# Chunked attention beside a bilinear layer: one TensorE visit per chunk, with two array modes in place of four

## The reference, cut to what matters

```python
# 1. gated linear attention; batch 4, heads 8, seq 768, head_dim 48
for t in range(S):
    state = alpha[:, :, t, :, None] * state + np.einsum('bhd,bhe->bhde', k[:, :, t], v[:, :, t])
    y[:, :, t] = np.einsum('bhd,bhde->bhe', q[:, :, t], state)
# 2. bilinear layer, 384 -> 1024 -> 384
x = ((x @ w1) * (x @ w2) @ w3) @ w_out
# 3. four experts, 384 -> 1024 -> 384, weighted by p
p = domain_probs / (domain_probs.sum(-1, keepdims=True) + 1e-09)
for e in range(E):
    out += p[:, e:e + 1] * (np.maximum(x @ w1[e], 0.0) @ w2[e])
```

## Time and profile before

| | |
|---|---|
| median of 3 runs | 1246.04 us (1245.34 to 1248.34) |
| profiled execution, its own time | 1246.21 us |
| its span | 1244.5 us |
| busy PE | 1238.9 us |
| busy DVE | 391.0 us |
| busy ACT | 285.2 us |
| busy POOL | 179.5 us |

### The profile page before, as it was taken

The page is one execution under the profiler, slowest core; times in us unless marked ns, Lnnn a source line. Parts: engine busy times, 40 slices in busy tenths (PEclk is TensorE's granted clock), DMA queues, the critical chain, the costliest instruction groups (busy, mean ns, idle before and its releaser), DMA issues.

```text
span 1244.5 us, 17887 instructions
## 1 busy us (share of the span) xinstructions
PE 1238.9 (100%) x7390; PEld 1119.1 (90%) x7390; DVE 391.0 (31%) x797; ACT 285.2 (23%) x554; POOL 179.5 (14%) x157
## 2 busy tenths in 40 slices
PE   9999999999999999999999999999999999999999
PEld 5699999999999999999999898999999998989998
DVE  4455454544643122222222222122222222222222
ACT  2433333333332421111111111111111111111111
POOL 1522222222222640000000000000000000000000
PEclk9999999999999999999999999999999999999999
DMA  9612323232322431111141111103111111222200
GB/s 280 202 54 87 93 83 106 69 106 69 106 76 94 155 141 51 51 51 51 51 152 52 52 51 51 46 23 135 52 51 51 51 51 51 77 76 76 76 16 36
DMA packets 41314, 99.57 MB, mean 80 GB/s; under 512 B 3360, under 2 KB 13344, under 8 KB 40736
## 3 DMA queue, kind: packets, MB, share of 16 engines
q1 hardware_dynamic: 41248, 98.63, 24.5%
HBM read 82.10 MB, written 14.16 MB: 77 GB/s over the span
## 4 chain that ended last, share of the span: by engine, by line
PE 95%; DMA 2%; DVE 1%; POOL 1%; SPq 1%; issue 0%; DVEq 0%
PE bank L847 30%; PE bank L849 29%; PE bank L848 29%; PE bank L869 2%; PE bank L900 2%; DMA inputs<-akq 1%; PE bank L906 1%; PE bank L882 1%; POOL wb_lo L398 1%; PE bank L856 1%; DMA wo_sb<-w_out 1%; PE bank L990 0%; DVE decay L639 0%; DVE suffix L626 0%; SPq L298 0%; SPq L307 0%
## 5 line engine op out<-in xcount | busy, mean ns | idle before, releaser
L686 DVE SCALAR_TENSOR_TENSOR h_lo<-bank,h_hi 128x512 fp32r<-128x512 f32 x192 | 132.7, 691 | 617.8 <-ACT h_hi L497 617.8
L497 ACT ACTIVATE h_hi<-bank 128x512 fp32r<-128x512 f32 x192 | 115.0, 599 | 663.9 <-PE bank L849 663.9
L848 PE MATMUL bank<-we_lo,h_hi 128*128 128x384 f32 x768 | 257.1, 335 | 0.0
L847 PE MATMUL bank<-we_hi,h_hi 128*128 128x384 f32 x768 | 257.0, 335 | 0.0
L849 PE MATMUL bank<-we_hi,h_lo 128*128 128x384 f32 x768 | 256.9, 335 | 0.0
L849 PE MATMUL bank<-x_hi,we_lo 128*128 128x512 f32 x576 | 228.1, 396 | 0.0
L848 PE MATMUL bank<-x_lo,we_hi 128*128 128x512 f32 x576 | 227.1, 394 | 0.0
L847 PE MATMUL bank<-x_hi,we_hi 128*128 128x512 f32 x576 | 226.4, 393 | 0.0
L847 PEld LDWEIGHTS bank<-we_hi,h_hi 128*128 128x128 f32 x768 | 144.3, 188 | 8.9 <-DVEq L835 0.4
L848 PEld LDWEIGHTS bank<-we_lo,h_hi 128*128 128x128 f32 x768 | 144.1, 188 | 8.8
L849 PEld LDWEIGHTS bank<-we_hi,h_lo 128*128 128x128 f32 x768 | 144.1, 188 | 0.0
(11 more groups left out here) (75 smaller groups left out, 1086.2 us busy)
## 6 DMA issues: line engine op xcount, KB each, us to landing
x_hi<-x_hi_spill SPq DMA_DIRECT2D x24, 768.0 KB, 4.9
x_lo<-x_lo_spill SPq DMA_DIRECT2D x24, 768.0 KB, 6.4
inputs<-akq SPq DMA_DIRECT2D x24, 672.0 KB, 5.6
we_raw<-wset SPq DMA_DIRECT2D x4, 3072.0 KB, 10.2
values<-v_rows SPq DMA_DIRECT2D x24, 256.0 KB, 5.5
x_hi_spill<-x_hi_out SPq DMA_DIRECT2D x8, 576.0 KB, 3.4
x_lo_spill<-x_lo_out SPq DMA_DIRECT2D x8, 576.0 KB, 4.6
w_sb<-w_t SPq DMA_DIRECT2D x16, 256.0 KB, 11.9
```

Of the source, the lines that this page charges most:

```text
L497: act.activation(h_hi[:, s % 2, :], bank[s % 2][:, :], ACT.Relu).then_inc(h_hi_ready, 1)
L686: dve.scalar_tensor_tensor(out=h_lo[:, s % 2, :], in0=bank[s % 2][:, :], scalar=0.0, in1=h_hi[:, s % 2, :], op0=ALU.max, op1=ALU.subtract) ...
L847: pe.matmul(dst, left[0], right[0], start=first, stop=False)
L848: pe.matmul(dst, left[0], right[1], start=False, stop=False)
```

## The change

Per chunk there is now one place on PE at which attention is worked, in the even step (`visit`), instead of two:

- it starts with the value products of chunk c (128x64), then the state products of chunk c+1 (128x64);
- then, in one 64x64 block, the state's share of the outputs of chunk c (`state_share`) mixed with the scores of chunk c+1 (`score`). A score matmul now has 64 keys as weights: the first 64 keys against all 128 queries, the last 64 keys against the last 64 queries only. That is 16 matmuls of 128 or 64 columns where 8 of 128 were;
- the outputs are all in bank 7, so the even heads' share must be complete before the odd heads' share starts (`even_shared`, a wait of PE for itself); the state products are in what is left of banks 5 and 6;
- `mask` is eight operations of 256 or 128 elements instead of two of 512; `add_state` is two instead of one; the x0 split is one instruction of 512 elements instead of two of 256 on ACT and on DVE;
- the preparation of a chunk is done one chunk further ahead, `turn_keys` stands behind `down1` of the odd step, and SP loads a chunk before it moves rows. A copy of the chunk's decay (`chunk_decay`) is added;
- in the start the visits stand at other places, visit 2 (which has the scores of chunk 3) among them; DVE prepares chunk 3 behind `take(0, 1)`, and two of the four parts of the first weight set are loaded after chunk 3's inputs.

```diff
             def mask(b, c):
-                for row in range(2):
-                    dve.tensor_tensor(scores[:, row, :, :], bank[5 + row][:, :]..., causal[:, None, :]..., ALU.mult).then_inc(masked, 1)
+                for row in (1, 0):
+                    dve.wait_ge(scored, 2 * (CHUNKS * b + c) + 2 - row)
+                    # four dve.tensor_tensor: 64 x 2x128, 64 x 2x64, 64 x 2x64, 64 x 2x128
+                last.then_inc(masked, 1)
...
+            def take(b, c):
+                x0_low(b, c)
+                first = chunk_behind(b, c)
+                if first:
+                    if first[1] >= 1:
+                        decay_state(*first)
+                    if first[1] < CHUNKS - 1:
+                        add_state(*first)
+                    mask(*first)
...
+            def state_share(b, c, row, n):
+                g, q = divmod(n, 2)
+                if row == 1 and n == 0:
+                    pe.wait_ge(even_shared, (CHUNKS - 1) * b + c)
+                rows = slice(row * ODD, row * ODD + D)
+                mm = pe.matmul(bank[7][q * ODD:(q + 1) * ODD, (2 * row + g) * CHUNK:(2 * row + g + 1) * CHUNK], decayed[rows, 2 * g + q, :],
+                               inputs[rows, c % SLOTS, Q, 2 * g + q, :], start=False, stop=(row == 1 and g == 1))
+                if n == PAIRS - 1:
+                    mm.then_inc(y_done if row else even_shared, 1)
+
+            def score(c, row, n):
+                pair, half = divmod(n, 2)
+                lower = (pair + half) % 2 == 0
+                at = pair // 2 * GROUP + (pair % 2) * (CHUNK if lower else HALF)
+                rows = slice(row * ODD, row * ODD + D)
+                mm = pe.matmul(bank[5 + row][0 if lower else HALF:HALF if lower else P, at:at + CHUNK - half * HALF],
+                               inputs[rows, c % SLOTS, K, pair, half * HALF:(half + 1) * HALF],
+                               inputs[rows, c % SLOTS, Q, pair, half * HALF:], start=True, stop=True)
...
+            def visit(b, c):
+                value_products(b, c)
+                first = chunk_behind(b, c)
+                if first and first[1] < CHUNKS - 1:
+                    state_products(*first)
+                if first:
+                    wait_scores(*first)
+                if c >= 1:
+                    pe.wait_ge(state_decayed, (CHUNKS - 1) * b + c)
+                if c >= 1 and first:
+                    for n in range(3 * PAIRS):
+                        if n < PAIRS:
+                            state_share(b, c, 0, n)
+                        else:
+                            score(first[1], 0, n - PAIRS)
+                        if n < 2 * PAIRS:
+                            score(first[1], 1, n)
+                        else:
+                            state_share(b, c, 1, n - 2 * PAIRS)
...
                     if chunk and s % 2 == 0:
-                        score(*chunk)
-                        if chunk[1] < CHUNKS - 1:
-                            state_products(*chunk)
-                    if chunk and s % 2:
-                        outputs(*chunk)
-                        if not (last_batch and chunk[1] == CHUNKS - 1) and chunk_behind(*chunk)[1] < CHUNKS - 1:
-                            turn_keys(*chunk_behind(*chunk))
+                        visit(*chunk)
...
                     down1(b, s)
+                    if chunk and s % 2:
+                        second = chunk_behind(*chunk, 2)
+                        if second and second[1] < CHUNKS - 1:
+                            turn_keys(*second)
...
-            first_beside = {3: ((turn_keys, 0),), 4: ((score, 0), (state_products, 0)), 5: ((outputs, 0), (turn_keys, 1)),
-                            6: ((score, 1), (state_products, 1)), 7: ((outputs, 1), (turn_keys, 2))}
-            second_beside = {2: ((score, 2), (state_products, 2)), 6: ((outputs, 2),), 20: ((turn_keys, 3),)}
+            first_beside = {3: (turn_keys, 0), 4: (first_visit, 0), 6: (turn_keys, 1), 7: (visit, 0)}
+            second_beside = {5: (turn_keys, 2), 9: (visit, 1), 15: (turn_keys, 3), 20: (visit, 2)}
...
             pe.wait_ge(fold_lo, FT - 1)
             pe.wait_ge(piece_lo, PIECES)
             up1(0, 0, 1, True)
+            turn_keys(0, 4)
```

More of the change, by code:

```diff
@@ L66 @@
 WARM = 6
-CONSTANTS = 6
+CONSTANTS = 7
 FLAG_STEP = STEPS1 - 4
-PREP_STEPS = 4
+PREP_STEPS = 5
+HALF = CHUNK // 2
+GROUP = 3 * HALF
+STATE_AT = 2 * GROUP
 REDO_ROWS = PAIRS * D
@@ L331, in _ @@
                 load_chunk(0, c + SLOTS)
+                move_rest(0, c)
+                if c == 0:
+                    for i in range(PARTS // 2, PARTS):
+                        load_part(i)
             sp.dma_start(gate[:, :, :], probs).then_inc(gate_loaded, 16)
@@ L501, in bilinear @@
                     chunk = chunk_beside(b, s, last_batch) if beside else None
+                    second = chunk_behind(*chunk, 2) if chunk else None
                     following = s + 1 < STEPS1 or (beside and not last_batch)
-                    prepares = chunk and not (last_batch and chunk[1] == CHUNKS - 1)
                     if following:
@@ L649, in add_state @@
+                last.then_inc(masked, 1)
             def add_state(b, c):
                 dve.wait_ge(state_added, (CHUNKS - 1) * b + c + 1)
[L652 to L655 removed]
+                dve.wait_ge(scored, 2 * (CHUNKS * b + c) + 2)
+                if c >= 1:
                     dve.wait_ge(state_decayed, (CHUNKS - 1) * b + c)
[L657 removed]
+                for half in range(2):
+                    pairs = slice(2 * half, 2 * half + 2)
+                    new = bank[5 + half][0:PD, STATE_AT:STATE_AT + 2 * D].rearrange("p (a e) -> p a e", a=2)
+                    if c == 0:
+                        last = dve.tensor_copy(state[:, pairs, :], new)
+                    else:
+                        last = dve.tensor_tensor(state[:, pairs, :], new, decayed[:, pairs, 0:D], ALU.add)
@@ L899, in outputs @@
                             at = slice((4 * g + 2 * q + row) * ODD, (4 * g + 2 * q + row + 1) * ODD)
-                            mm = pe.matmul(bank[7 - row][q * ODD:(q + 1) * ODD, g * CHUNK:(g + 1) * CHUNK], values[:, c % SLOTS, at],
-                                           scores[:, row, 2 * g + q, :], start=(g == 0), stop=(c == 0 and g == 1))
-                for g in range(2 if c >= 1 else 0):
-                    for row in range(2):
-                        for q in range(2):
-                            rows = slice(row * ODD, row * ODD + D)
-                            mm = pe.matmul(bank[7 - row][q * ODD:(q + 1) * ODD, g * CHUNK:(g + 1) * CHUNK], decayed[rows, 2 * g + q, :],
-                                           inputs[rows, c % SLOTS, Q, 2 * g + q, :], start=False, stop=(g == 1))
@@ L908, in outputs @@
-                mm.then_inc(y_done, 1)
+                            mm = pe.matmul(bank[7][q * ODD:(q + 1) * ODD, (2 * row + g) * CHUNK:(2 * row + g + 1) * CHUNK], values[:, c % SLOTS, at],
+                                           scores[:, row, 2 * g + q, :], start=(row == 0 and g == 0), stop=(c == 0 and row == 1 and g == 1))
+                if c == 0:
+                    mm.then_inc(y_done, 1)
+            def state_share(b, c, row, n):
[7 more added lines that the diff above has]
+                    mm.then_inc(y_done if row else even_shared, 1)
@@ L994, in _ @@
                     pe.wait_ge(constants, CONSTANTS)
-                for step, c in first_beside.get(k, ()):
+                if k in first_beside:
+                    step, c = first_beside[k]
                     step(0, c)
@@ L1006, in _ @@
                     mm.then_inc(folded, 1)
-                for step, c in second_beside.get(n, ()):
+                if n in second_beside:
+                    step, c = second_beside[n]
                     step(0, c)
```

209 lines of the change are left out of this document (105 added, 104 removed).

## The result

The changed kernel took 1248.07 us (median of 20 runs, 1246.83 to 1252.58), the kernel before 1245.93 in the same comparison (20 runs): a ratio of 1.0016, 95% interval 1.0008 to 1.0023. The span of the profiled execution is 1245.6 us, 1.1 more than before.

The account below looks back on a forecast made before the run. PE was taken to bound the kernel, busy 1238.9 of 1244.5 us. A bilinear-layer gain of -13.7 and a start loss of +3.3 sum to -10.4 us, from 1246.2 to 1236 us; range 1232 to 1243.

Parts of the forecast that it names:

- the walk through DVE's order: In the start, DVE's operations listed up to chunk 3's keys, ready at 48.9; PE wants them at 45.5.
- The visits: Attention on PE, bilinear layer: full visit 3.03 us, chunk 4 without state products 2.57, chunk 0 without share 2.52, transposes 0.42.
- 0.07 for `even_shared`: PE's added wait in the middle of the 64x64 block: 0.07 us, zero if the release is quicker.
- In step: Rival for the 64x64 block: a 64-column pass costs as much as its 128-column neighbour; 1240 us, chance 0.22.
- two at a time: Rival for the 64x64 block: passes run two side by side, 56 ns each; 1266 us, chance of slower 0.06.
- The last visit: Bilinear layer, the visit with nothing behind it: 1.82 us on PE.
- All of it is hidden: Bilinear layer: DVE's 4.1 us after a visit fits before `g_product` at 4.7, so other engines' work costs nothing.
- Masks: DVE's eight masks per chunk: 0.33 us for 256 elements, about 0.2 for 128, 2.1 together.
- The wait at chunk 3: In the start, PE stands 3.4 us before chunk 3's transposes, until DVE has the keys.
- Experts and PE's clock are as they were: Whole kernel: no change in time from the experts or from PE's clock.
- the start: Up to the second `up1`, near 64.5 against 61.24: loses 3.3 us, bounds 1.5 and 5.
- the bilinear layer: Attention on PE there falls from 79.5 to 65.8 us, a gain of 13.7.

Follow-up runs that it names:

- experiment 7: Changed kernel with four of the eight masks left out (last 64 keys with last 64 queries): 1239.85 us, ratio 0.9942.
- experiment 8: Changed kernel with a start order keeping DVE and POOL apart, and bilinear-layer transposes moved between the halves of the next up1: 1239.66 us, ratio 0.9934.
- experiment 4: Changed kernel plus six unused products on PE ahead of the wait for chunk 3's keys, so PE is not idle: 1246.16 us, ratio 0.9997.
- Experiment 9: As experiment 8, plus one line: POOL waits for DVE's decay of the state for chunk 2 before its last ten pieces: 1236.59 us, ratio 0.9917.
- experiment 10: As Experiment 9, but DVE prepares chunk 4 ahead of taking chunk 2: 1240.45 us, ratio 0.995.
- experiment 3: Changed kernel, but DVE prepares chunk 3 ahead of taking chunk 1 instead of behind it: 1248.49 us, ratio 1.0008.
- experiment 1: Changed kernel with a new start order: DVE folds a piece first, prepares chunks 3 and 4 earlier; PE's visits later; ACT and SP follow: 1243.71 us, ratio 0.9979.
- experiment 6: As experiment 3, but POOL scales chunk 3's queries ahead of all pieces of wb_lo, so it is idle while DVE scans: 1243.46 us, ratio 0.9981.
- experiment 2: Changed kernel with only PE's places moved: transposes of chunk 3 behind product 20, visit 2 behind 22: 1244.81 us, ratio 0.9987.

## Why the prediction was wrong

The step that failed is the walk through DVE's order. The prediction had DVE late at one place, for 3.4 us, and "hidden, at no cost" everywhere else. The profile has PE waiting for it for 0.40, 2.49, 4.24 and 1.37 us in the start and just behind it, and for 0.65 us three times later. PE's clock, which was to be as before, was low behind the longest of these waits.

- **The visits: right.** 3.00, 2.56, 2.50 and transposes of 0.40 against 3.03, 2.57, 2.52 and 0.42. The block took 1.33 us against 1.27 + 0.07 for `even_shared`. "In step" and "two at a time" did not come about.
- **The last visit: mis-sized.** 2.53 for 1.82 (+0.7). There are no scores to put between the even and the odd share, so the wait for `even_shared` is bare. I gave it the price of the old outputs, which used two banks and had no such wait.
- **"All of it is hidden" in the bilinear layer: wrong.** I compared DVE's 4.1 us after the visit with `g_product` 4.7 us after it, and did not list the other things that wait for the masks. The transposes of the next chunk do, one `down1` after the next `up1`; in three batches a split of `x1` (1.49 us) had pushed DVE back, and PE stood 0.65 us and paid a second entry: 3 x 0.84. Experiments 7 and 8 took these three waits away in two different ways. In the same stretch four scans took 2.32 us in place of 1.6 and the decay 1.08 in place of 0.35, beside POOL; that alone is more than the wait, and no experiment took it apart from the masks. The first batch lost 2.0 more, at the last piece of the fold behind the preparation of chunk 4, which the late start had put beside POOL's pieces (scans 2.34 us in place of 1.37, clamp 1.22 in place of 0.42).
- **Masks: mis-sized**, 2.9 us for 2.1, and by a slip and not for want of rows. The line through 192 elements in 0.35 us and 512 in 0.645 gives 0.41 for 256 and 0.29 for 128, not 0.33 and 0.2. Measured are 0.41 to 0.43 and 0.28 to 0.30. With the right reading DVE is done 4.8 us after a visit, and `g_product` is possible after 4.7: the cover would have been gone on paper.
- **The wait of 2.49 us at chunk 2's transposes: missing.** I walked through DVE's order for chunk 3 alone. The same masks stand ahead of chunk 2's transposes five products into the fold.
- **The wait at chunk 3: right in kind**, 4.24 for 3.4, the difference being the masks. **What comes behind it: wrong.** "Experts and PE's clock are as they were" held for the experts; in the start the clock fell behind the wait, some 2.3 us (experiment 4). POOL's `wb_lo`, forecast at 64.3, came at 71.6, since it hangs on ACT, and ACT on the late visit.
- Of the 7.2 us by which the start missed, 2.5 are the wait at chunk 2, 0.8 the longer wait at chunk 3, some 2.3 the clock. About 1.0 lies ahead of all this: 0.65 in the first 14 us (the fold goes on at 14.26 behind a wait for a load, before at 13.61) and a wait of 0.40 at chunk 1's transposes. The last 0.6 I did not place.
- In sum the start was forecast at +3.3 and was +10.5; the bilinear layer at -13.7 and was -9.3. Experiment 9, which takes the waits away and keeps the visits, gives 1236.6. So the cost of the new work on PE was right, and the cost of being late was not. That experiment 9 lands on the forecast of 1236 is in part luck: its start costs 2.0 and its bilinear layer gains 11.2, where 3.3 and 13.7 were forecast.

## What to carry to other kernels

When a change gives a helper engine more and smaller operations, list every instruction of the main engine that waits for the last of them, at each place in the program, and walk through the order of the helper for each; its busy share tells nothing. Price an idle main engine above its idle time, for the clock behind it may fall. Before work is moved into idle time of DVE, look at what POOL does in that time.

## What the runs showed of the hardware that was not expected

**DVE and POOL hold each other up.** DVE operations on SBUF stretched beside POOL's (four scans 4.57 us against 1.60; a copy of four elements 0.96 against 0.14; a decay of 192 elements 0.92 to 1.44, once 8.34, against 0.35). Not all did: the reciprocal kept its 0.18 beside the ten pieces of experiment 10. Masks and splits, which read PSUM, kept their 0.28, 0.42 and 0.66 (experiment 9). POOL pays as well: beside the scaling of the keys on DVE its first two pieces in experiment 3 took 3.17 us in place of 2.50. The Trainium skill, "SBUF — State Buffer", section "SBUF: two separate sides", has the rule: a DVE instruction with two inputs in SBUF, or in a mode that uses both ports, shares a pair of ports with GpSimd, and whichever starts first keeps it for its whole instruction. The runs agree for the scans, which took about one of POOL's pieces each (4.57 us for four, a piece 1.24). They go beyond it in one point: the decay of experiment 8 ended only behind a whole row of POOL's instructions, not behind one. In the changed kernel the decays of the bilinear layer are long too, 16 of 17, each beside POOL's `scale_queries` (L415). POOL starts that when the scans have ended, and the new order has the decay just behind them; before, all of them took 0.35. A view that groups DVE's instructions by line, 72 to 400 us (count, busy us, mean ns), then one decay in time order and what POOL does beside it:

```profile
L690 DVE TENSOR_TENSOR decayed<-state,chunk_decay 112x192 f32<-112x192 f32 x17 | 16.8, 990 | 0.0
...
178.78 1.08 DVE L690 TENSOR_TENSOR decayed<-state,chunk_decay 112x192 f32<-112x192 f32 x1
...
178.35 1.29 POOL L415 TENSOR_TENSOR inputs<-inputs,decay 112x512 f32<-112x512 f32 x1 [1.11 <-DVE decay L653]
```

**The clock.** After an idle time of 4.24 us (and 4.97, 5.26, 5.59 and 6.32 in experiments 1, 8, 3 and 10) PE's products ran at half rate, and the low clock went on for 3.8 to 5.6 us in which PE was busy. It fell after 3.03 us in experiment 7 and 2.25 in experiment 6 too. After some waits it went both ways: not after 2.49 us in the changed kernel, but after the same 2.49 us in experiment 4; not after 1.37 us in the changed kernel, but after the same 1.37 us in experiment 2. What decides between these I did not find out. A wait of PE of 1.4 us or more can cost as much again behind it.

**Small tiles.** 48 passes of 64x64 weights start 24 ns apart over four tiles and three banks. The Trainium skill, "TensorE: Matmul & The Clock Gate", Part 3, says that matmuls start and end strictly in the order of the program. Here passes of 64 columns do not take the time of their 128-column neighbours: a block in step would have needed 1.3 us in place of 1.1. Nor do the records start in the order of the program. When the eighth and last pass of the even share starts (175.79), 17 passes of the block have started; in the program it is the fourteenth. So the rule does not hold between tiles here. The ends are modelled in this profile and decide nothing.
